# One half block's layer input made in PSUM, filler transposes on TensorE, and the near score entries by matmul, in a two-layer kernel behind a linear attention

## The reference

```
for t in range(768):                       # 4 batches, 8 heads, head size 48
    cur = u[None] * k_t (outer) v_t
    y_t = r_t . (state + cur)
    state = w_t * state + k_t (outer) v_t
x = y as (3072, 384)
x = (sigmoid(x @ w_gate) * (x @ w_val)) @ w_out          # 384 -> 1536 -> 384
x = elu(x @ w_in) @ w2_out                               # 384 -> 2048 -> 384
```

## Time and profile before

| | us |
|---|---|
| median of 3 runs | 1090.01 (1088.66 to 1096.51) |
| the profiled execution | 1089.36 |
| its span, first to last instruction | 1087.6 |
| PE busy | 1050.8 (97% of the span) |
| DVE, ACT, POOL busy | 614.3, 481.1, 239.9 |
| DMA, mean rate | 47 GB/s |

### The profile page before, as it was taken

How to read it: one execution, slowest core, us unless ns; L and a number is a source line. 1 busy time by engine, 2 the same in 40 slices (tenths; PEclk the granted TensorE clock), 3 DMA queues, 4 the chain that set the end, 5 groups by cost and what they waited for, 6 DMA issues and landing times.

```text
span 1087.6 us, 20585 instructions
## 1 busy us (share of the span) xinstructions
PE 1050.8 (97%) x8380; PEld 911.3 (84%) x8380; DVE 614.3 (56%) x916; ACT 481.1 (44%) x903; POOL 239.9 (22%) x255
## 2 busy tenths in 40 slices
PE   5888899999999999999999999999999999999998
PEld 5778888787878787888788888899999999989998
DVE  6777986769386848674866333534334343333433
ACT  2646435343333343334334333645445454444543
POOL 8141743434243415351442000000000000000000
PEclk9999999999999999999999999999999999999999
DMA  7653450413152114312300422301001010010000
GB/s 134 119 135 90 81 71 20 67 26 46 34 66 40 32 42 58 52 19 57 43 5 2 126 67 63 98 1 58 1 1 58 1 58 1 1 60 1 30 1 30
DMA packets 146654, 51.48 MB, mean 47 GB/s; under 512 B 116352, under 2 KB 144256, under 8 KB 146560
## 3 DMA queue, kind: packets, MB, share of 16 engines
q1 hardware_dynamic: 146560, 50.16, 22.6%
HBM read 39.52 MB, written 9.44 MB: 45 GB/s over the span
## 4 chain that ended last, share of the span: by engine, by line
PE 86%; DVE 6%; issue 2%; DMA 2%; SPq 2%; ACT 1%; POOL 0%; DVEq 0%; POOLq 0%
PE ps L762 25%; PE ps L797 18%; PE ps L789 18%; PE ps L772 12%; PE ps L700 4%; PE ps L663 3%; PE ps L721 2%; PE ps L728 2%; PE ps L706 1%; DVE A L1086 1%; DVE A L1090 1%; DVE hl L1144 1%; DVE RKW L1018 1%; DVE work L1156 1%; PE ps L736 1%
## 5 line engine op out<-in xcount | busy, mean ns | idle before, releaser
L762 PE MATMUL ps<-xh,WS 128*128 128x512 f32 (+1 forms) x1008 | 254.4, 370 | 9.9 <-DVE WS L1166 7.1
L818 ACT ACTIVATE hh<-work 128x512 fp32r<-128x512 f32 (+1 forms) x180 | 108.5, 603 | 228.3 <-DVE work L1156 146.3
L762 PEld LDWEIGHTS ps<-xh,WS 128*128 128x128 f32 x1008 | 171.7, 190 | 40.0 <-DVE WS L1166 8.5
L797 PE MATMUL ps<-WS,hh 128*128 128x384 f32 x768 | 195.5, 335 | 0.6 <-DVE hl L1140 0.6
L789 PE MATMUL ps<-xh,WS 128*128 128x512 f32 x576 | 161.3, 392 | 0.0
L772 PE MATMUL ps<-hh,WS 128*128 128x512 f32 (+1 forms) x504 | 158.9, 370 | 0.8 <-DVE hl L1144 0.8
L1183 DVE SCALAR_TENSOR_TENSOR work<-work,ps 128x512 f32<-128x512 f32 x96 | 65.9, 687 | 165.3 <-ACT work L962 165.3
L585 POOL TENSOR_TENSOR RKW<-RKW,WL 128x256 f32<-128x256 f32 x144 | 120.1, 852 | 145.1 <-PE ps L700 96.3
L797 PEld LDWEIGHTS ps<-WS,hh 128*128 128x128 f32 x768 | 139.8, 188 | 8.0 <-DVE hl L1140 1.1
L762 PE MATMUL ps<-xl,WS 128*128 128x512 f32 (+1 forms) x504 | 131.6, 369 | 0.0
L797 PE MATMUL ps<-WS,hl 128*128 128x384 f32 x384 | 128.8, 335 | 0.0
(11 more groups left out here) (80 smaller groups left out, 1266.1 us busy)
## 6 DMA issues: line engine op xcount, KB each, us to landing
nat<-in_w_dram SPq DMA_DIRECT2D x24, 192.0 KB, 3.9
nat<-in_r_dram SPq DMA_DIRECT2D x24, 192.0 KB, 4.7
nat<-in_k_dram SPq DMA_DIRECT2D x24, 192.0 KB, 5.3
V<-in_v_dram SPq DMA_DIRECT2D x24, 192.0 KB, 4.8
x_scratch<-work SPq DMA_DIRECT2D x12, 384.0 KB, 3.3
nat<-x_scratch SPq DMA_DIRECT2D x6, 768.0 KB, 6.4
out_dram<-A SPq DMA_DIRECT2D x5, 768.0 KB, 4.3
RKW<-in_moe_w_in_dram SPq DMA_DIRECT2D x16, 192.0 KB, 2.4
```

Source lines behind the costliest of these rows:

```text
L762: last = mm(val(m, j) if second else ps[:, GATE, t], gate_w(a, second, j, c), xp[b][:, c, t], start=(i == 0 and c == 0), stop=(i == 2 and ...
L797: last = mm(ps[:, ACC2 + b, 0:HD], hp[ap][:, j % 2, b * P:(b + 1) * P], down2_w(wp, j), start=(j == 0 and i == 0), stop=(j == F2 - 1 and i ...
L818: return nc.scalar.activation(o, i, ACT.Copy)
```

## The change

For q = 0 the stages become Tw, Tr, Tk, L1, L2, L3, N, L4, L5, L6, KT, Z, S, X; for q = 1 a stage N comes after L3; later halves are as before.

N makes the near entries of block 0 on PE. ACT makes two more copies of r and k from PSUM (`near_part`): in the copy of r the even steps, in that of k the odd ones are scaled by u, head by head. 32 matmuls of 64 by 64 then give the diagonal (with u) and the entry beside it (without), and DVE copies them into A by a mask in 8 masked copies per half (`near_sums`). POOL's products, DVE's sums and the second load of r are gone for q = 0 and 1. The copies of r and k lie in buffers that stand free then (prod, shift, ub, xs); so u on all partitions is loaded later, after q = 1's N, and `shift` is cleared by POOL at q = 1's KT.

X makes q = 0's x in PSUM. Z computes the part on other partitions, ACT copies it to y3 (`a_last`), and X adds it with a matmul by a placing matrix `put` to the other parts of A times v. `move_y(0)` and Y of q = 0 are gone, and ACT and DVE split x right out of PSUM. The copies of ST follow behind that.

Filler transposes of the identity (`turn_unit`) are issued on PE in q = 0: 14 before Tw, 2 before Tr, 2 before Tk, then 6, 0, 10, 10, 10, 5 before L1 to L6, 4 before Z. In front of L they are issued as soon as the stage's PSUM banks are free, ahead of the waits for r and k. Their results are never read.

q = 1's Tr comes after ("x", 0) and the first gate step. Loads of half 1 no longer wait for POOL's products.

```diff
+    FIRST = STAGES[:NEAR_AT] + ["N"] + STAGES[NEAR_AT:-2] + ["Z", "S", "X"]
+    SECOND = STAGES[:NEAR_AT] + ["N"] + STAGES[NEAR_AT:]
...
-    LEAD = len(PARTS[0]) + 4
-    PROGRAM = USES[:LEAD] + [("x", 0)]
+    LEAD = len(PARTS[0]) + 2
+    PROGRAM = PARTS[0] + [("x", 0)] + USES[len(PARTS[0]):LEAD]
...
-    EARLY = {("a", 0, "KT", 1): 2, ("x", 0): 2, ("a", 1, "Tk", 0): 2}
+    EARLY = {("a", 0, "Z", 1): 2, ("x", 0): 2, ("a", 1, "Tr", 0): 2}
...
             load_half(0)
-            load_shift(0)
-            sp.dma_start(ub[:], u.rearrange("h d -> (h d)").partition_broadcast(P)).then_inc(u_loaded, 16)
+            sp.wait_ge(d_zero, 5)
+            for e in range(2):
+                sp.dma_start(u_rows[e * HP:e * HP + D], u.rearrange("(p e) d -> e d p", e=2)[e],
...
-            load_shift(1)
-            move_y(0)
...
             load_shift(2)
+            sp.wait_ge(s_att, count("a", 1, "N", 1))
+            sp.dma_start(ub[:], u.rearrange("h d -> (h d)").partition_broadcast(P)).then_inc(u_loaded, 16)
             move_y(1)
...
-            FIRST_TERMS = {(0, "L1", 1): "rk", (0, "L2", 1): "u", (0, "L3", 1): "r'k",
-                           (1, "L3", 1): "rk", (1, "L4", 1): "u", (1, "L5", 1): "r'k",
-                           (2, "L1", 1): "rk", (2, "L2", 1): "u", (2, "L3", 1): "r'k"}
+            FIRST_TERMS = {(2, "L1", 1): "rk", (2, "L2", 1): "u", (2, "L3", 1): "r'k"}
...
+            IDLE = {1: 6, 2: 0, 3: 10, 4: 10, 5: 10, 6: 5}
+
+            def turn_unit(bank, times):
+                for _ in range(times):
+                    nc.tensor.transpose(bank[:, 0:P], ident[:], ident[:])
...
                         if b == 0 and q == 0:
+                            turn_unit(ps[:, GATE, :], {"Tw": 14, "Tr": 2, "Tk": 2}[name])
                             pe.wait_ge(d_zero, STAGES.index(name) + 1)
...
+                elif name == "N":
...
+                    pe.wait_ge(a_near, near_operand(q, "Tk", b))
+                    for g in pairs:
+                        for own in (slice(0, HP), slice(HP, P)):
+                            for e in range(2):
+                                rows = slice(e * HP, (e + 1) * HP)
+                                last = mm(heads[e][own, g * HP:(g + 1) * HP], slot(near_k[b], g % PR)[rows, own],
+                                          slot(near_r[b], g % PR)[rows, own], start=True, stop=True)
...
+                            if q == 0:
+                                turn_unit(heads[0], IDLE[li])
+                        pe.wait_ge(d_r, scaled(q, li - 1, b))
+                        pe.wait_ge(p_k, level(q, li - 1, b))
...
+                elif name == "X":
+
+                    pe.wait_ge(a_put, 1)
+                    pe.wait_ge(a_last, 1)
+                    for c in range(KC):
+                        for x in range(U):
+                            mm(x_sums(c)[:, x * P:(x + 1) * P], put[:, c, :], y3[:, x, :], start=(x == 0), stop=False, skip_group_check=True)
+                        for x in range(U):
+                            for e in range(2):
+                                last = mm(x_sums(c)[e * HP:e * HP + D, x * P:(x + 1) * P], V[:, hf, x * PR + c, e, :],
+                                          A[:, x * PR + c, e, :], start=False, stop=True, skip_group_check=True)
...
+                for at, run in runs:
+                    copy(run.rearrange("p g (i two) -> p g i two", two=2)[:, :, :, plain], src[:, at:at + run.shape[1], :, plain])
+                for p in range(PR):
+                    last = nc.scalar.activation(slot(runs, p).rearrange("p (i two) -> p i two", two=2)[:, :, with_u],
+                                                src[:, p, :, with_u], ACT.Copy, scale=u_rows[:, p:p + 1])
...
+                    if q == 0 and (name, b) == ("Tk", 1):
+                        for tname in ("Tr", "Tk"):
+                            for x in range(U):
+                                near_part(q, tname, x)
+                    elif q == 1 and name in ("Tr", "Tk"):
+                        near_part(q, name, b)
...
+                if m == 0:
+                    for c in range(KC):
+                        if c < KC - 1:
+                            act.wait_ge(s_x, c + 1)
+                        else:
+                            act.wait_ge(s_att, count("a", 0, "X", 0))
+                        copy(xh[:, c, t], x_sums(c)).then_inc(a_xhi, 1)
+                    copy_state(0)
+                    return
...
+            def near_sums(q, b):
...
+                for own in (slice(0, HP), slice(HP, P)):
+                    for e in range(2):
+                        last = nc.vector.copy_predicated(
+                            A[own, b * PR:(b + 1) * PR, e, own],
+                            near_mask[own].bitcast(I32).unsqueeze(1).to_broadcast([HP, PR, HP]),
+                            ps[own, at[e], b * PR * HP:(b + 1) * PR * HP].rearrange("p (g t) -> p g t", g=PR))
```

More of the change, by code:

```diff
@@ L365, in masked, with near_operand, slot @@
             return q * sum(TILES.values()) + sum(TILES[x] for x in TILES if x <= li)
+        def near_operand(q, name, b):
+            return 4 * q + {"Tr": 0, "Tk": 2}[name] + b + 1
+        def slot(runs, p):
+            return [run[:, p - at] for at, run in runs if 0 <= p - at < run.shape[1]][0]
         def w1_raw(x):
@@ L406, in load_shift @@
                 n, hf = q // HALF, q % HALF
[L408 to L410 removed]
+                if q == HALF:
+                    sp.wait_ge(p_zero, 7)
+                wait(sp, d_dots, carried(q))
                 for b in range(U):
@@ L818, in copy, with near_part @@
                 return nc.scalar.activation(o, i, ACT.Copy)
+            def near_part(q, name, b):
+                if (q, name, b) == (0, "Tr", 0):
+                    act.wait_ge(u_rows_loaded, 32)
+                src = ps[:, bank_of("a", q, name, b), :].rearrange("p (g i two) -> p g i two", g=PR, two=2)
+                runs = (near_r if name == "Tr" else near_k)[b]
+                plain, with_u = (1, 0) if name == "Tr" else (0, 1)
+                for at, run in runs:
[3 more added lines that the diff above has]
+                                                src[:, p, :, with_u], ACT.Copy, scale=u_rows[:, p:p + 1])
+                last.then_inc(a_near, 1)
             def attention(q, name, b):
@@ L872, in attention @@
                         last.then_inc(a_rp, 1)
-                elif name == "Y":
+                elif name == "Z" and b == 1:
+                    act.wait_ge(d_zero, 9)
+                    act.wait_ge(s_att, count("a", q, name, b))
+                    for e in range(2):
+                        rows = slice(e * HP, e * HP + D)
+                        last = copy(y3[rows], ps[rows, bank_of("a", q, name, b), 0:U * P].rearrange("p (b t) -> p b t", b=U))
+                    last.then_inc(a_last, 1)
+                elif name == "Y" and q > 0:
                     act.wait_ge(s_att, count("a", q, name, b))
@@ L1133, in split_y @@
                 t = cols(m)
+                if m == 0:
+                    for c in range(KC):
+                        dve.wait_ge(a_xhi, c + 1)
+                        tt(xl[:, c, t], x_sums(c), f32(xh[:, c, t]), ALU.subtract).then_inc(d_xlo, 1)
+                    return
                 for c in range(KC):
@@ L1202, in _ @@
             nc.vector.reduce_sum(even, ident[:, 0:P:2], axis=AX.X).then_inc(d_zero, 1)
+            dve.wait_ge(p_masks, 2 * NM)
+            dve.wait_ge(d_zero, 7)
+            for own, pairs in ((slice(0, HP), slice(0, HP // 2)), (slice(HP, P), slice(HP // 2, HP))):
+                to = near_mask[own].rearrange("p (i two) -> p i two", two=2)
+                nc.vector.tensor_scalar(to[:, :, 0], masks[own, 0, pairs], even[own], None, ALU.mult).then_inc(d_near_mask, 1)
+                nc.vector.tensor_copy(to[:, :, 1], masks[own, 0, pairs]).then_inc(d_near_mask, 1)
+            nc.vector.memset(put, 0.0).then_inc(d_zero, 1)
+            nc.vector.memset(y3[:], 0.0).then_inc(d_zero, 1)
             for step in PROGRAM:
```

147 lines of the change are left out of this document (100 added, 47 removed).

## The result

| | before | after |
|---|---|---|
| median, us | 1089.7 (1088.31 to 1096.51, 20 runs) | 1095.2 (1093.44 to 1100.8, 20 runs) |
| the profiled execution, us | 1089.36 | 1094.19 |
| its span, us | 1087.6 | 1092.4 |

The ratio after to before is 1.0042, 95% interval 1.0029 to 1.0055. By this ratio the kernel became slower by about 4.6 us (the medians differ by 5.5). I had forecast 1085.4 and a range of 1079.5 to 1090.5: the sign was wrong and the time lies outside the range. A slowdown of 0.42% still falls under "within 1%", which had 0.87.

A forecast was written before the change was run, and what follows sets the result against it. PE bounds the kernel from 160 us on; from 41 to 105 us SP paces it, with DVE and ACT. 1089.36 less 3.1 (SP) and 1.0 (waits, stretched splits) gives 1085.3, stated as 1085.4; range 1079.5 to 1090.5.

The forecast's parts named there:

- The copy of `put` on ACT is done before the first bank of Tw (6.4), within 0.1 us.: At the start of q = 0, ACT's added copy of the placing matrix delays the Tw copies by at most 0.1 us.
- the 1.15 us by which Tk and L1 were to end sooner: Early in q = 0, PE at full clock ends Tk and L1 1.15 us sooner than before.
- at Tr or Tk: Where in q = 0's start PE was to get its full clock, eight transposes then taking about 1.1 us.
- rival 3: In q = 0 the fillers run at half clock, third xh copy at about 45, split 9 at 60; 1097 us, chance 0.08.
- the case that I had placed between rival 3 and the forecast: In q = 0 the clock rises only about L4; time between 1097 and 1085.4 us, no chance of its own.
- X: 1.5 us forecast: At q = 0's X, six placing matmuls at 0.11 and twelve of A times V at 0.068 make 1.5 us.
- The lead at x: Third xh copy of q = 0 over at 33.0 in place of 41.0, 8.0 us sooner.
- ACT from x to split 9: ACT's work between third xh copy and split 9, 14.7 us with 5.2 of near copies; split 9 ends at 47.7.
- Now piece 13 can go out directly behind piece 12, at about 50.0: SP is 3.7 us ahead.: On SP's queue, L1's masks of q = 1 no longer hold piece 13; 3.7 us ahead, 3.1 after u's load.
- my sum: Lead up to q = 1's move_y: 3.1 us on SP's queue plus 1.0 from waits and stretched splits.
- the ring: From 41 to 105 us PE waits for splits, splits for DMAs, DMAs for SP; about 2 us of waits after 53.7.

The follow-up runs named there:

- e7_nofill: e5_old1 without any filler transposes; 1088.21 us, ratio to before 0.9985.
- e4_no_fill: The kernel after with no filler transposes; 1094.49 us, ratio to before 1.0039.
- e6_fill2: e5_old1 with 6, 8, 0, 0, 8, 0 fillers ahead of L1 to L6; 1087.84 us, ratio to before 0.9985.
- e11_before_fill: The kernel before with only the fillers ahead of Tw to Tk and L1 to L6 added; 1088.68 us, ratio to before 0.9995.
- e3_no_near1: The kernel after without ACT's near copies for q = 1 (near entries there not the reference's); 1092.67 us, ratio to before 1.0036.
- e2_late: The kernel after with q = 1's N and near copies moved behind L6; 1093.82 us, ratio to before 1.0033.
- e10_best_nofill: e7_nofill with w of half 2 loaded behind pieces 12 and 15, not 10 and 11; 1086.85 us, ratio to before 0.9983.
- e5_old1: The kernel after with q = 1's near entries made as before and the near mask built at q = 0's L4; 1090.68 us, ratio to before 1.0006.
- e8_between: The kernel after with w of half 2 loaded behind pieces 12 and 15, not 10 and 11; 1096.18 us, ratio to before 1.0068.

## Why the prediction was wrong

The ratios from after to e7_nofill fall by 0.0057 in all (6.2 us), which is well clear of noise: 0.0017 with the mended start, 0.0019 with q = 1's near entries as before, 0.0021 without the fillers. What is left of the change, x in PSUM and N for q = 0, gains 0.0015 (1.6 us). The three shares go by the order of the edits and are each uncertain by about 0.0017. Taken from after one at a time, q = 1's near entries were worth 0.0014 and the fillers 0.0003. So the start and q = 1 are shown as causes, of about 2 us each, and the fillers are not.

1. **"The copy of `put` on ACT is done before the first bank of Tw (6.4), within 0.1 us."** This step failed first. The copy came at 10.03, since the two DVE instructions ahead of its source were stretched to the end of POOL's clearing at 9.06. I priced the copy and not what it was queued behind. With it went the 1.15 us by which Tk and L1 were to end sooner: L1 began at 13.88, before at 13.02.
2. **The clock.** It rose within Tw (8 in 1.41), sooner than my "at Tr or Tk", and was not held: down at L2, so the ten fillers ahead of L3 cost 2.37 and not 1.1. This is rival 3's mechanism for one level, and then the clock rose in L3 and stayed up for N and L4, the case that I had placed between rival 3 and the forecast. L6 was over at 31.3, not 26.5.
3. **A rule of the Trainium skill** (TensorE: Matmul & The Clock Gate, Part 4: PE-mode transpose) says that the full clock doesn't engage for transposes. The traces disagree: in e4_no_fill PE did nothing but transposes up to 12.0 us and went from 1.94 to 1.07 for eight. Rival 3 hung on that rule. Why the clock fell again is not shown: in after it fell by L2 behind gaps of 1.21 and 1.27 us in PE's work, in e6_fill2 it stayed up over one of 1.75 us, and in e11_before_fill it was down with PE 8.95 of 10 us busy.
4. **X: 1.5 us forecast, 3.7 measured, mostly by a miscount.** I took "6 x 0.11 + 12 x 0.068", matmuls of the code times prices per row of the profile, but a plain fp32 matmul is two rows: X has 12 rows of placing and 24 of A times V. By the starts of the rows an A times V row takes 0.073 us, as priced, so that term is 1.7 and not 0.8. A placing row takes 0.16, and a placing matmul thus 0.32 where I had 0.11, at most 0.14, by the transpose; that term is 1.9 and not 0.7. N has 64 rows too, where I had 32; they took 1.1 us at the full clock, so its 1.2 was right by luck. S, forecast beside X, ran in the wait for y3's copy and cost nothing, but the four fillers ahead of Z cost 0.6. near_sums took 3.29 against 3.1, well priced, but from 31.2 and not from 26.5.
5. **The lead at x: 8.0 us forecast, 0.1 measured.** near_sums ended at 34.5 and not at 29.6: 4.9 us by steps 1 and 2. X's end came at 40.5 and not at 32.5, 3.1 us more: 2.2 by X, 0.6 by Z's fillers. With the start mended and the fillers gone (e7_nofill) the lead is 3.5.
6. **ACT from x to split 9: right in the total, not in the share of the near copies.** 14.7 forecast, 13.7 measured, with one gap of 0.7. The scaled copies of 64 elements came at 0.20 us each, as estimated. But I had added the near copies whole, 5.2 us, and the stretch is only 2.5 shorter without them (11.1, e3_no_near1), as ACT then waits for DVE. The other 3.9 us over the 7.3 of before stay without them; no run takes them apart. With a lead of 0.1 in place of 8.0 all of it was paid: split 9 is 6.3 us later than before.
7. **"Now piece 13 can go out directly behind piece 12, at about 50.0: SP is 3.7 us ahead."** It did go out directly (57.08 behind 55.28), but piece 12 was 5.8 us later than before. From split 9 (6.3 late) to x1 (4.8 late) 1.5 us came back, where my sum had 3.5 (0.6 of lead at split 9, 4.1 at the end).
8. **Not in the prediction at all:** N's PSUM bank, which L4 of q = 1 takes again, so that PE stands 4.54 us behind DVE's near copies. I costed the copies as DVE's time and didn't ask which bank they hold. As e2_late shows, it matters little in the end.
9. **What the path looks like once there is a lead.** e7_nofill had x0 3.5 us ahead, split 9 0.3 behind and x1 2.2 ahead. That is the forecast's shape in small: the lead at x is gone by split 9, and 2.6 us come back behind it, 2.1 of them already at piece 13, which L1's masks no longer hold up. It is one profile, and the stretch from split 9 to x1 is not steady: 56.3 us in before and 54.5 in e11_before_fill, whose code is the same there. DVE is at its limit around the splits: busy 6.92 of 7 us from 48 to 55 before, 6.91 in e10_best_nofill. Which step of the ring decides after 55 us stays open.

What stays open too: how much of the remaining 1.6 us is x in PSUM and how much is N for q = 0, as no run had one without the other; where e6_fill2 and e7_nofill got their 2.3 us over e5_old1; and the disagreement in e3_no_near1. The fastest version, e10_best_nofill at 0.9983, is not told apart from e7_nofill.

## What to carry to other kernels

Price an added set-up instruction by what it is queued behind and by what runs beside it on POOL, not by its size: two copies of 64 by 32 elements and a copy queued behind them cost 2 us of the kernel here. Take a price and a count from the same list: rows of the profile times the price of a row, or matmuls of the code times the price of a matmul. No run here became faster by fillers. Fillers to raise TensorE's clock must fall into waits that they don't lengthen, and they can pay only where TensorE's pace is what the next engine waits for; look for that before adding any. When work is moved from a waiting engine to one that is full later (here ACT between x and split 9), the lead that is to pay for it must be there first; test the lead by itself.

## What the runs showed of the hardware

- Small DVE instructions from SBUF to SBUF lasted until POOL's clearing was over: 64x32 in 3.95 and 3.82 us beside three MEMSETs, 0.24 and 0.18 behind them. Five decay steps took 3.34 us beside POOL's products of k, 1.18 to 1.19 alone.
- TensorE's clock can rise over nothing but transposes (8 in 1.94, 1.77, 1.07 in e4_no_fill), and doesn't in every execution: in e7_nofill, with the first two eights at nearly the same times (5.41 and 7.83 against 5.33 and 7.74), all three took 1.94.
- The clock column does not show this: it read 1.00 from 0 to 25 us in before and in e7_nofill, where the eights took 1.94.
- The granted clock can fall while PE is loaded with fillers: 0.50 from 15 to 25 us in e11_before_fill, with PE busy 8.95 of 10 us. The same PE code lost it ahead of L1 in one execution (e8_between) and by L2 in another (after).
- A plain fp32 matmul shows as two rows of the profile, a transpose as one. By the starts of the rows, at the full clock, a matmul of 128 columns with a 128 by 128 weight took 0.32 us and a transpose of that size 0.11.
